# Gate-folding products spread singly among the expert-layer tiles, one y in a bank of its own, and one GpSimd step behind a VectorE step

## The reference

```
# 1. attention with a state that decays (batch 4, 8 heads, 768 steps, head width 48)
y_t   = r_t @ (state + (u*k_t) v_t^T)
state = w_t * state + k_t v_t^T
# 2. dense layer, 384 -> 2048 -> 384
h = x @ w_in;  g = h * tanh(softplus(h));  x2 = g @ w_out
# 3. routing over 8 experts, 384 tokens each, in the order of the largest logits,
#    and one small two-layer network per expert
logits = x2 @ w_gate;  out[mask_e] = relu(x2[mask_e] @ w1[e]) @ w2[e]
```

## Time and profile before

| | |
|---|---|
| median of 3 runs | 848.12 us (845.80 to 849.88) |
| the profiled execution | 849.38 us, span 847.6 us |
| TensorE, VectorE busy | 802.7 us (95%), 641.2 us (76%) |
| ScalarE, GpSimd busy | 405.4 us (48%), 282.4 us (33%) |
| mean granted TensorE clock | 0.968 of full speed |

### The profile page before, as it was taken

One profiled execution on the slowest core, in us unless ns is written; L12 is line 12 of the kernel. 1 busy time (PEld: TensorE's weight loads), 2 busy tenths in 40 slices (PEclk: granted clock), 3 DMA queues, 4 the chain that ended last, 5 costly groups with the idle time before them and its releaser, 6 DMA issues. The chain is left out here.

```text
span 847.6 us, 16953 instructions
## 1 busy us (share of the span) xinstructions
PE 802.7 (95%) x6744; PEld 596.4 (70%) x6744; DVE 641.2 (76%) x1123; ACT 405.4 (48%) x655; POOL 282.4 (33%) x244
## 2 busy tenths in 40 slices
PE   8999999999999999999898999986799999999995
PEld 8888878787878787868676777754465665666662
DVE  8879788898979897979696987767768677776220
ACT  2457557575767667575756476920112211212221
POOL 3315262534444443444251625001212312313311
PEclk9897999999999999999999999998599999999999
DMA  9952236363545445463817354103324244235410
GB/s 312 334 193 61 72 125 249 105 243 125 218 155 201 173 168 207 140 232 120 315 59 289 121 182 136 75 20 131 139 106 177 68 167 178 89 146 205 190 43 29
DMA packets 47790, 133.48 MB, mean 157 GB/s; under 512 B 5344, under 2 KB 19808, under 8 KB 45664
## 3 DMA queue, kind: packets, MB, share of 16 engines
q1 hardware_dynamic: 38880, 93.07, 31.2%
q0 software_dynamic: 5376, 34.61, 11.1%
q10 hardware_dynamic: 3456, 4.72, 1.5%
HBM read 97.78 MB, written 34.60 MB: 156 GB/s over the span
## 5 line engine op out<-in xcount | busy, mean ns | idle before, releaser
L413 PE MATMUL bank<-x_hi,win_hi 128*128 128x256 f16 x576 | 160.5, 279 | 0.0
L413 PE MATMUL bank<-x_lo,win_hi 128*128 128x256 f16 x576 | 160.3, 278 | 0.0
L413 PE MATMUL bank<-x_hi,win_lo 128*128 128x256 f16 x576 | 160.1, 278 | 0.0
L1438 POOL TENSOR_TENSOR g_lo<-t_sb,g_hi 128x512 f16<-128x512 f32 x88 | 117.4, 1355 | 82.0 <-ACT g_hi L726 82.0
L413 PE MATMUL bank<-wout_hi,g_hi 128*128 128x392 f16 (+1 forms) x416 | 129.5, 318 | 0.8 <-issue 0.8
L413 PE MATMUL bank<-wout_lo,g_hi 128*128 128x392 f16 (+1 forms) x416 | 129.2, 317 | 0.0
L413 PE MATMUL bank<-wout_hi,g_lo 128*128 128x392 f16 (+1 forms) x416 | 129.1, 317 | 0.0
L1422 POOL TENSOR_TENSOR dv<-v_tok,dot 128x384 f32<-128x384 f32 x24 | 39.6, 1649 | 210.3 <-DVE dot L948 210.3
L726 ACT ACTIVATE g_lo<-bank 128x384 f16<-128x384 f32 x64 | 31.4, 490 | 144.5 <-PE bank L413 144.5
L726 ACT ACTIVATE g_hi<-t_sb 128x512 f16<-128x512 f32 x96 | 56.8, 624 | 89.1 <-DVE t_sb L995 65.9
L995 DVE TENSOR_TENSOR t_sb<-t_sb,h_sb 128x512 f32<-128x512 f32 x96 | 89.8, 964 | 5.4 <-ACT t_sb L726 3.4
(11 more groups left out here) (179 smaller groups left out, 1514.0 us busy)
## 6 DMA issues: line engine op xcount, KB each, us to landing
stage<-in_moe_w SPq DMA_DIRECT2D x32, 768.0 KB, 6.7
w_split<-stage SPq DMA_DIRECT2D x32, 768.0 KB, 5.3
wt<-in_w_turned SPq DMA_DIRECT2D x24, 258.0 KB, 5.3
kt<-in_k_turned SPq DMA_DIRECT2D x24, 256.0 KB, 4.8
rt<-in_r_turned SPq DMA_DIRECT2D x24, 256.0 KB, 5.2
r_tok<-in_r SPq DMA_DIRECT2D x24, 192.0 KB, 6.5
k_tok<-in_k SPq DMA_DIRECT2D x24, 192.0 KB, 6.8
v_tok<-in_v SPq DMA_DIRECT2D x24, 192.0 KB, 4.8
```

The costliest lines, as they stand in the source:

```text
L413: return nc.tensor.matmul(*a, **k)
L1438: G.tensor_tensor(g_lo[:, j * GW:(j + 1) * GW], t_sb[:, j * GW:(j + 1) * GW], g_hi[:, j * GW:(j + 1) * GW], ALU.subtract).then_inc(s["glo" ...
```

## The change

- The 48 fold products are no longer made in four groups of 12. A tile issues one fold product behind the second of every three of its own products: 6 each in tiles 4 to 7 of turn 0, 4 each in tiles 0 to 5 of turn 1. Tile (0, 4) now waits for the loads of the fold's operands. ScalarE's rounding of the result goes from slot 4 to slot 6 of turn 1, VectorE's remainder from slot 6 to slot 7.
- Chunk 1's y and its turned x go to bank `ab[1]`, so `values(1)` no longer waits for `xhi` and `xlo` of chunk 0; 3 filler products stand ahead of it.
- GpSimd's `diagonal(1)` waits for VectorE's second `rdec`.

```diff
+        def y_bank(n):
+            return ab[1] if n == 1 else Y
...
-                pe.wait_ge(s["xhi"], n)
-                pe.wait_ge(s["xlo"], n)
+                if n > 1:
+                    pe.wait_ge(s["xhi"], n)
+                    pe.wait_ge(s["xlo"], n)
...
+            to_fold = [(t, k3) for t in range(FT) for k3 in range(KT)]
+            FOLDS = {**{(0, j): 6 for j in range(4, NJ)}, **{(1, j): 4 for j in range(6)}}
+
+            def fold_one():
+                t, k3 = to_fold.pop(0)
+                q, f = t // (FT // 4), t % (FT // 4)
+                last = mm(ab[0][:, t * E:(t + 1) * E], wot[q][:, k3, f * P:(f + 1) * P], w_gate[:, k3, :],
+                          start=k3 == 0, stop=k3 == KT - 1)
+                if f == FT // 4 - 1 and k3 == KT - 1:
+                    last.then_inc(s["fold"], 1)
...
+                folds = FOLDS.get((i, j), 0)
+                if (i, j) == (0, 4):
+                    pe.wait_ge(s["gload"], 16)
+                    pe.wait_ge(s["wotload"], 64)
...
                     for t, (a, b) in enumerate(ops):
                         last = mm(hb[HB[j]][:, f * TOK:(f + 1) * TOK], a, b, start=t == 0, stop=t == len(ops) - 1)
+                        if folds and t % 3 == 1 and 3 * f + t // 3 < folds:
+                            fold_one()
...
-                        folded([0])
                         scores(2)
...
-                        folded([1])
...
-                if i == 1 and slot in (1, 2):
-                    folded([slot + 1])
...
             keys(1)
+            warm(ident[:, :], 3)
             values(1)
...
-                if i == 1 and slot == 4:
+                if i == 1 and slot == 6:
                     act.wait_ge(s["fold"], 4)
...
-                    if i == 1 and slot == 6:
+                    if i == 1 and slot == 7:
                         dve.wait_ge(s["foldhi"], 1)
...
             own(0)
+            pool.wait_ge(s["rdec"], 2)
             diagonal(1)
```

More of the change, by code:

```diff
@@ L444, in values @@
                     pe.wait_ge(s["state"], with_keys(n))
-                pe.wait_ge(s["xhi"], n)
-                pe.wait_ge(s["xlo"], n)
+                if n > 1:
+                    pe.wait_ge(s["xhi"], n)
+                    pe.wait_ge(s["xlo"], n)
                 pe.wait_ge(ld["v"][c], 16 * (n // CH + 1))
+                y = y_bank(n)
                 for q in range(NQ):
                     if not first_of(n):
-                        mm(Y[:, 2 * q * D:(2 * q + 2) * D], rdec[c][:, q, :], state[:, q, :], start=True, stop=False)
+                        mm(y[:, 2 * q * D:(2 * q + 2) * D], rdec[c][:, q, :], state[:, q, :], start=True, stop=False)
                     for h in (2 * q, 2 * q + 1):
-                        last = mm(Y[:, h * D:(h + 1) * D], att[:, h, :], v_tok[c][:, h, :],
+                        last = mm(y[:, h * D:(h + 1) * D], att[:, h, :], v_tok[c][:, h, :],
                                   start=first_of(n), stop=first_of(n) or h % 2 == 1)
@@ L466, in turn_x @@
                 for k3 in range(KT):
-                    last = nc.tensor.transpose(Y[:, k3 * P:(k3 + 1) * P], x_tok[c][:, k3 * P:(k3 + 1) * P],
+                    last = nc.tensor.transpose(y_bank(n)[:, k3 * P:(k3 + 1) * P], x_tok[c][:, k3 * P:(k3 + 1) * P],
                                                ident[:, :])
                 last.then_inc(s["xT"], 1)
+            to_fold = [(t, k3) for t in range(FT) for k3 in range(KT)]
[7 more added lines that the diff above has]
+                    last.then_inc(s["fold"], 1)
             def tile(i, j):
@@ L538, in finish @@
                 pass
[L540 to L549, removed]
             def turn(i, slot):
@@ L739, in turn_x @@
                     act.wait_ge(s["h"], NJ * (i - 1))
-                A(x_hi[i % 2][:, :, c * P:(c + 1) * P], Y[:, 0:DM].rearrange("p (k t) -> p k t", k=KT),
+                A(x_hi[i % 2][:, :, c * P:(c + 1) * P], y_bank(n)[:, 0:DM].rearrange("p (k t) -> p k t", k=KT),
                   scale=SX).then_inc(s["xhi"], 1)
@@ L954, in sum_x @@
                     dve.wait_ge(s["xT"], n - 1)
-                V.tensor_tensor(x_tok[n % CH][:, :], Y[:, 0:DM], dv[:, :, :].rearrange("p h d -> p (h d)"),
+                V.tensor_tensor(x_tok[n % CH][:, :], y_bank(n)[:, 0:DM], dv[:, :, :].rearrange("p h d -> p (h d)"),
                                 ALU.add).then_inc(s["x"], 1)
@@ L981, in low_x @@
                 V.scalar_tensor_tensor(x_lo[i % 2][:, :, c * P:(c + 1) * P],
-                                       Y[:, 0:DM].rearrange("p (k t) -> p k t", k=KT), SX,
+                                       y_bank(n)[:, 0:DM].rearrange("p (k t) -> p k t", k=KT), SX,
                                        x_hi[i % 2][:, :, c * P:(c + 1) * P], ALU.mult, ALU.subtract
```

## The result

| | before | changed |
|---|---|---|
| median of 5 runs | 847.96 us (845.61 to 849.88) | 852.56 us (850.86 to 854.93) |
| ratio, 95% interval | | 1.0051 (1.003 to 1.0072) |
| timed again, 12 runs | 847.53 us | 849.56 us (845.36 to 855.84), ratio 1.0013 (0.9995 to 1.0032) |
| profiled execution, span | 849.38, 847.6 us | 850.86, 849.1 us |

The changed kernel is slower in the first comparison; in the second its interval includes 1, so it can't be told from the kernel before. The forecast, 846.4 us within 842.3 to 849.6, was wrong in sign. The profiled execution of the changed kernel is the fastest of its first five runs, so its 1.5 us of extra span show only a part of the loss.

The account below looks back on a forecast made before the run. TensorE, busy 802.7 of 847.6 us, was taken as the bound. Prologue gain, folds and low clock brought sums(0, 0), the line, from 99.8 to 98.1; that 1.7 us, carried unchanged, gave 846.4 us, range 842.3 to 849.6.

Parts of the forecast that it names:

- The prologue's walk: Steps up to tile (0, 0): waits removed, clock stays up, `state` slow at 1.9 us, tile starting at 28.55.
- The forecast 1.3 us: Gain at the start of tile (0, 0): 28.55 where it was 29.88.
- the split ends at 39.3: Turn 0, VectorE: the split needed by tile (0, 4) ends at 39.3 where it ended at 40.95.
- tiles (0, 4) and (0, 5) at full clock, 6.6 us: Turn 0, TensorE: these two tiles with 12 folds take 6.6 us and end at 45.9, against 48.34.
- about 1.3 for a low clock behind the wait: Turn 1: time added from tile (1, 3) on because a wait of nearly 5 us leaves the clock down.
- my 19.7: Tile (1, 3) to sums(0, 0): 15.8 us at full clock, 2.6 for 12 folds, about 1.3 for low clock.
- My bound: Behind the wait ahead of tile (1, 3): clock up gives 1.3 us more gain, down twice as long 1.5 less.
- the clock could stay low in tiles with folds: Objection set aside: 18 of the 30 instructions there are full tile products, where the groups had none.
- the gain is eaten: Rival: `state` clash and longer low clock behind the wait leave no gain, 848.1 us; chance 0.18 with nothing changed.
- the clock falls somewhere else as often: Rival that the change does nothing it says; time as the eaten gain, 848.1 us; the two share chance 0.18.
- 0.22, bounded from 0.11 to 0.34: Cost in us of a single fold between tile products, 36 on the path; the bounds give gains 5.7 and -2.6.
- dear folds: Rival: precision changes stall TensorE at single folds; at 0.42 us each the time is 853.6 us; chance 0.07.

Follow-up runs that it names:

- diag_only: The kernel before with only GpSimd's `diagonal(1)` wait for VectorE's second `rdec` added: 846.48 us, ratio 0.9992.
- spread_only: The kernel before with only the spread folds and moved roundings, without the new bank, fillers and GpSimd wait: 849.97 us, ratio 1.0025.
- spread_again: The same kernel as `spread_only`, timed once more beside `spread_tail`: 848.16 us, ratio 1.0018.
- spread_tail: `spread_only` with the 12 folds of tiles (1, 3) to (1, 5) in a group behind tile (1, 2): 847.63 us, ratio 0.9999.
- late_low: The changed kernel with GpSimd's `win_lo` waiting for VectorE's second split: 845.11 us, ratio 0.9984; timed again 849.04 us, ratio 1.0004.
- late_tail: `late_low` with the 12 folds of tiles (1, 3) to (1, 5) grouped behind tile (1, 2): 845.10 us, ratio 0.998; again 844.62, 0.997.
- both_guards: `late_tail` with GpSimd's `diagonal(2)` also waiting for VectorE's `state` of chunk 1: 845.52 us, ratio 0.998.

## Why the prediction was wrong

**The prologue's walk was right, its gain was in part luck of the one trace.** `scores(1)` lost its wait, `values(1)` started at 21.38 (21.7), `state` took 2.13 beneath `diagonal(2)` (1.9), tile (0, 0) started at 28.87 (28.55), and the clock stayed up at 24.6. But the low stretch of 24.6 to 31.4 is not in every execution with chunk 1's y in the common bank: of its seven profiles, the clock was up there in four (`diag_only`, `spread_only`, `spread_again`, `spread_tail`), and tile (0, 0) then started at 28.35 to 28.82, no later than in the changed kernel (28.49 to 28.87). In these four the split and GpSimd's `win_lo` also start within 0.1 us of each other, so the toss comes without the new bank, and what the new bank adds is GpSimd's lead. The forecast 1.3 us was a gain over executions like the one that I had read.

**The step that failed first:** the walk along VectorE's chain from `x_lo(1)` to "the split ends at 39.3". It ended at 42.31. VectorE did work without a pause, but one link of the chain took 4.59 us where I had carried over its 1.73. I moved VectorE's chain and TensorE's, but not ScalarE's and GpSimd's with them: `x_hi(1)` came 2.3 us earlier than before, `win_lo` on GpSimd with it, and it fell on the split. I had weighed just such an overlap for `state`, under 4 us ahead of the place where it cost more. The experiments show that its price depends on what covers it: with groups of folds nothing that can be measured (847.26 with the clash, 846.51 without), with spread ones tile (0, 4) starts 2.8 us later (42.41 against 39.59 in `late_low`). I had counted the group ahead of `scores(2)` as work removed, not as cover for a late `rdec`. I had also put tiles (0, 4) and (0, 5) at full clock, 6.6 us; they took 8.38 with the clock down in the first profile of the changed kernel. In the second they took 5.60: it waited 1.59 and 0.58 us just ahead of them, and its low stretch lay earlier, from 29.6 to 33.0. So those two waits alone do not bring the clock down, and what does is not shown.

**The second step that failed:** "about 1.3 for a low clock behind the wait". That wait came, 2.31, 3.92 and 5.54 us in the three profiles. In the first the stretch from tile (1, 3) to the line took 101.25 - 82.07 = 19.2 us, for my 19.7. In the second tile (1, 3) started at 78.91, for my 78.35, and only then was the gain lost: 102.19 - 78.91 = 23.3. In the third it took 105.44 - 81.62 = 23.8. My bound allowed for a low clock of twice 3.4 us; it lasted 13.7 and 17.1. I had also set aside, in one sentence, that the clock could stay low in tiles with folds, because most of their instructions are full products. It did, in seven of nine profiles for longer than 3.4 us, and with the folds moved ahead of these tiles in none of six; how much of that is the folds' doing and how much the wait's is open, as said above. The rival "the gain is eaten" named the longer low clock behind the wait, but gave it "0.4 or more". The prediction's list of low stretches also lacks one of the kernel before, 75.8 to 79.2, in which TensorE ran slowly just ahead of this place; no term of the sum was taken from it. The rival that the clock falls somewhere else as often came near, too: from 14 us to the line the changed kernel's three profiles have 17.0, 20.5 and 23.9 us at 1.2 GHz, that of the kernel before 23.9.

**A term mis-sized the other way.** A single fold at full clock took (57.57 - 54.77 - 1.97)/6 = 0.14 us, where 1.97 is a bare tile (54.29 - 52.32 before). I took 0.22, bounded from 0.11 to 0.34. On 36 folds that is 2.9 us in favour of the change, and with it the walk would have said 4.6 us faster. `late_tail`, in which neither loss was seen, was 2.0 and 2.6 us faster than the kernel before by its medians.

**What held.** The chain from tile (0, 7) to VectorE's copy moved with its start (3.4 and 3.1 us later than before), the moved roundings stopped nothing on TensorE (VectorE waited 1.47 us for the fold's rounding ahead of its remainder), and the two spans behind the line are equal. I had given 0.06 to slower by over 0.5%. The first comparison came out there, at 0.51%, and the second did not; of the mechanism that I had for it, dear folds, nothing was seen.

**What stays open.** The first comparison gave 0.51% and the second 0.13%, with intervals that barely meet. Two causes, each of which takes hold in some runs and not in others, make such a spread, but that the shares differed between the two comparisons is not shown. From the line to the end of the span the profiles of this case take 746.9 to 749.9 us, and that part of the spread was not looked into.

## What to carry to other kernels

When an instruction comes earlier, move every engine that it releases, and look for what the newly moved one runs beside: here a ScalarE rounding, three steps from the edit, started GpSimd on top of VectorE. Before small work is spread or removed, ask what lateness of another engine it covered. And try small work inside a wait rather than among the products behind it: here only the two versions with the 12 folds in the wait and GpSimd's `win_lo` held back (`late_tail`, `both_guards`) had an interval below 1. Last, a low stretch of clock in one trace need not be in the next: what a change gains by removing it should be read from several.

## What the hardware showed that was not expected

- Two elementwise instructions with both inputs in SBUF (the on-chip memory), one on VectorE and one on GpSimd, did not share evenly: one ran near its own pace and the other took nearly both times. VectorE 1.73 with GpSimd 4.59 to 4.73, or VectorE 4.58 to 4.63 with GpSimd 3.09 to 3.65, where alone they took 1.73 and 3.10 (`late_low`). With starts under 0.12 us apart it went either way; with GpSimd over 0.5 us ahead VectorE was the slow one in all five profiles.
- Behind a wait of 3.92 us TensorE stayed at 1.2 GHz for 13.7 us while busy in 12.3 of them, in tiles where an fp32 product of 8 columns stood behind one of every three products or fewer. In the six profiles with plain products there it was back after 3.4 us, but five of these had no wait ahead.
- An fp32 product of 8 columns took 0.14 us alone between fp16 products of 256 columns and 0.22 us in a group of its kind.
